# Eight columns instead of four in each group of a four-pass matmul order (gated scan and ELU feed-forward, fp32r)

## The reference

```
f = lower_bound + (1.0 - lower_bound) * sigmoid(f_logit)
i = 1.0 - f
for t in range(S):                       # S = 6080
    h = f[:, t] * h + i[:, t] * x[:, t]
    y[:, t] = h
h = y.reshape(B * S, 256) @ w_in         # 256 x 2048
g = where(h > 0, h, exp(min(h, 0)) - 1)
out = g @ w_out                          # 2048 x 256
```

## Time and profile before

| | before |
|---|---|
| median of 3 runs | 976.56 us |
| the profiled execution, its own time | 976.51 us |
| its span, from the first to the last instruction | 974.6 us |
| matmuls (PE) | 969.0 us busy, 4362 instructions |
| weight loads (PEld) | 815.1 us busy, 4362 instructions |
| VectorE (DVE) | 724.4 us busy |
| ScalarE (ACT) | 790.7 us busy |
| GpSimd (POOL) | 630.6 us busy |
| granted TensorE clock | 1.00 (2.4 GHz) |

### The profile page before, as it was taken

One profiled execution on the slowest core, in us unless ns is written; L12 is line 12 of the kernel. 1 busy time (PEld: TensorE's weight loads), 2 busy tenths in 40 slices (PEclk: granted clock), 3 DMA queues, 4 the chain that ended last, 5 costly groups with the idle time before them and its releaser, 6 DMA issues.

```text
span 974.6 us, 15016 instructions
## 1 busy us (share of the span) xinstructions
PE 969.0 (99%) x4362; PEld 815.1 (84%) x4362; DVE 724.4 (74%) x916; ACT 790.7 (81%) x1424; POOL 630.6 (65%) x477
## 2 busy tenths in 40 slices
PE   9999999999999999999999999999999999999998
PEld 6998888888888888888888888888888888888887
DVE  6987876976886796697688679678758867956444
ACT  7988878878888887887887888788788788787775
POOL 2587796576667667557656755856775765676544
PEclk9999999999999999999999999999999999999999
DMA  7212012002101201100210210120021021001001
GB/s 269 67 32 93 0 34 65 34 1 77 54 1 54 76 1 43 54 32 2 74 54 0 65 65 0 45 67 17 22 64 43 0 75 54 0 0 46 1 1 44
DMA packets 23078, 42.02 MB, mean 43 GB/s; under 512 B 2560, under 2 KB 4096, under 8 KB 23040
## 3 DMA queue, kind: packets, MB, share of 16 engines
q1 hardware_dynamic: 22752, 41.10, 13.1%
q10 hardware_dynamic: 288, 0.46, 0.2%
HBM read 29.10 MB, written 12.45 MB: 43 GB/s over the span
## 4 chain that ended last, share of the span: by engine, by line
PE 99%; DMA 0%; DVE 0%; ACT 0%; issue 0%; DVEq 0%
PE acc L898 17%; PE acc L897 17%; PE acc L899 17%; PE h L868 14%; PE h L867 14%; PE h L866 14%; PE h L1004 1%; PE h L1003 1%; PE h L1002 1%; DMA opening<-first_gate 0%; PE h L969 0%; PE h L979 0%; PE acc L1002 0%; PE acc L1003 0%; PE acc L1004 0%; DVE x L628 0%
## 5 line engine op out<-in xcount | busy, mean ns | idle before, releaser
L336 POOL TENSOR_TENSOR g_lo<-e,g_hi 128x512 fp32r<-128x512 f32 (+1 forms) x384 | 517.3, 1357 | 338.0 <-ACT g_hi L480 337.0
L466 ACT ACTIVATE e<-h 128x512 f32<-128x512 f32 (+1 forms) x379 | 225.1, 594 | 138.5 <-PE h L868 109.9
L719 DVE SCALAR_TENSOR_TENSOR e<-e,h 128x512 f32<-128x512 f32 (+1 forms) x379 | 256.6, 677 | 70.5 <-ACT e L472 69.8
L897 PE MATMUL acc<-g_hi,w_out_hi 128*128 128x512 f32 (+1 forms) x768 | 293.7, 382 | 0.0
L898 PE MATMUL acc<-g_lo,w_out_hi 128*128 128x512 f32 (+1 forms) x768 | 293.7, 382 | 0.0
L899 PE MATMUL acc<-g_hi,w_out_lo 128*128 128x512 f32 (+1 forms) x768 | 293.7, 382 | 0.0
L472 ACT ACTIVATE e<-e 128x512 f32<-128x512 f32 (+1 forms) x384 | 241.4, 629 | 9.8 <-issue 1.4
L480 ACT CAST g_hi<-e 128x512 fp32r<-128x512 f32 (+1 forms) x384 | 232.2, 605 | 18.3 <-DVE e L719 18.3
L866 PE MATMUL h<-a_hi,w_in_hi 128*128 128x512 f32 x616 | 236.6, 384 | 0.0
L868 PE MATMUL h<-a_hi,w_in_lo 128*128 128x512 f32 x616 | 236.6, 384 | 0.0
L867 PE MATMUL h<-a_lo,w_in_hi 128*128 128x512 f32 x616 | 236.5, 384 | 0.0
(11 more groups left out here) (77 smaller groups left out, 560.3 us busy)
## 6 DMA issues: line engine op xcount, KB each, us to landing
opening<-forget_logit SPq DMA_DIRECT2D x44, 256.0 KB, 2.6
x<-value SPq DMA_DIRECT2D x44, 256.0 KB, 2.7
out<-out_sb SPq DMA_DIRECT2D x44, 256.0 KB, 2.0
w_in_raw<-w_in SPq DMA_DIRECT2D x8, 256.0 KB, 5.4
w_out_raw<-w_out SPq DMA_DIRECT2D x8, 256.0 KB, 6.7
out<-out_sb SPq DMA_DIRECT2D x4, 224.0 KB, 2.0
x<-value SPq DMA_DIRECT2D x3, 224.0 KB, 6.0
opening<-forget_logit SPq DMA_DIRECT2D x2, 224.0 KB, 6.0
```

The costliest lines, as they stand in the source:

```text
L336: nc.gpsimd.tensor_tensor(g_lo[:, t % RING, 0:w], e[:, t % TILES, 0:w], g_hi[:, t % RING, 0:w].bitcast(F32), ALU.subtract).then_inc(g_lo_r ...
L466: nc.scalar.activation(e[:, i, 0:w], bank_of(j, t)[:, 0:w], ACT.Relu, scale=-1.0).then_inc(r_ready, 1)
L719: nc.vector.scalar_tensor_tensor(e[:, t % TILES, 0:w], e[:, t % TILES, 0:w], -1.0, bank_of(j, t)[:, 0:w], ALU.add, ALU.max).then_inc(g_rea ...
L897: nc.tensor.matmul(bank, hi, g_h, start=opens, stop=False)
```

## The change

The number of columns of a group goes from four to eight. The four passes stay, so a pass now takes columns 0 to 7, 32 to 39, 64 to 71, ..., the next 8 to 15, 40 to 47, and so on: 4 passes x 16 groups x 8 columns. The row holds the same 512 columns (2048 bytes) as before; a group is 32 bytes in place of 16, and the distance between the groups of a pass is 128 bytes in place of 64.

```
-LINE = 4
+LINE = 8
 APART = 4
 ...
 def in_order(columns):
     return columns.rearrange("p (b a c) -> p a b c", a=APART, c=LINE)
```

## The result

The changed kernel takes **963.62 us** (median of 4 runs, 963.19 to 963.72) against 976.59 us (976.37 to 976.63) of the kernel before. The ratio is 0.9867, with a 95% interval of 0.985 to 0.9884: 1.3% faster. The forecast was 989.7 us, slower, with a range of 966 to 1005 us. The time lies outside the range, and the direction was wrong.

The account below looks back on a forecast made before the run. TensorE was taken as the bound, without idle time. The profiled 976.5 us plus 3960 matmuls at 3.3 ns more each, 13.2 us, gave 989.7 us (+1.35%), with an 8-in-10 range of 966 to 1005 us.

Parts of the forecast that it names:

- What bounds the kernel: Whole kernel: TensorE has no idle time, so time changes by 3960 times the change of one distance between matmul starts.
- The upper end: Blocks 1 to 11: the new distance is bounded above by straight order's 230.0 ns, +6.7 ns a matmul, +26.4 us.
- Steps to the neighbouring group cost: Blocks 1 to 11: 64 of 127 steps go to neighbouring 16-byte groups, losing half the gain: +3.3 ns, +13.2 us; chance 0.30.
- The rival "no change": Blocks 1 to 11: the new order keeps 223.3 ns a matmul, 976.5 us within 0.2%; chance 0.27.
- The rival "faster": Blocks 1 to 11: 64 fewer jumps at 0.060 ns each, −3.8 ns a matmul, −15.2 us, 961.3 us; chance 0.23.
- The rival "all lost": Blocks 1 to 11: weight-load conflict returns, distance as in straight order, 230.0 ns, +26.4 us, 1002.9 us; chance 0.20.
- The 448-column stretch: Block 0: its 202.7 ns distance is near the 187 ns of a weight load, so may be bound by that.
- The rules: Memory rules: SBUF's makes groups of four and eight equal, 976.5 us; PSUM's favours fewer jumps; the trace was put above both.

Follow-up runs that it names:

- e1: Changed kernel with all matmuls of blocks 1 to 11 in straight order, 512 columns from first to last: 989.59 us.
- e8: Changed kernel with 36 series of 24 matmuls of 512 columns behind its end, each in one order, fp32r or bf16: 1167.39 us in all.
- e5: Changed kernel with groups of 8 in four passes on the moving row only, output written in straight order: 963.38 us.
- e6: Changed kernel with the moving row read in straight order and only the output in groups of 8 in four passes: 990.00 us.
- e7: Changed kernel with 64 bytes of room ahead of the rounded rows, so the moving rows begin 64 bytes further on: 989.15 us.
- e11: Changed kernel with the rounded rows put 512 bytes further on, a control for the shift by 64 bytes: 963.74 us.
- e9: Changed kernel with 28 series of 36 matmuls behind its end: fewer weight columns, other groups and passes, shifted moving rows: 1197.46 us in all.
- e14: Changed kernel with one extra matmul of 256 columns just before the first matmul of block 2: 1002.66 us.
- e2: Changed kernel with groups of 16 columns in four passes, 31 jumps: 1040.80 us.
- e4: Changed kernel with groups of 8 columns in two passes in place of four, 63 jumps: 1012.46 us.
- e3: Changed kernel with groups of 8 columns in eight passes in place of four, 63 jumps: 1016.74 us.

## Why the prediction was wrong

**What bounds the kernel: right.** TensorE without a gap, no instruction moved, cost = 3960 x the change of one distance. Span and distance agree within 0.5 us.

**The upper end: off.** 230.0 ns for the straight order came from eight distances in the opening. As a steady stream it has 226.7 ns (e1); a fresh series has more at first, 24 matmuls of e8 give (5.64 − 0.38) / 23 = 229 with their beginning. That the stretch was short stood in the text; the number was used all the same.

**"Steps to the neighbouring group cost": the step that failed.** It made the new order an interpolation between two known ones, 3.3 ns above groups of 4. The measured distance is 3.3 ns below them, 220.0 and not 226.6 ns. Groups of 16 have still more such steps than groups of 8 and should have been between them and the straight order; they have 239.5 ns, 12.8 above it. Groups of 8 in two and in eight passes have just as many as in four and run at 232.4 and 233.3. The distance is no monotonic function of group, jumps or passes: it goes with the order in which the moving row is read (e5, e6), with where the row begins (e7, e11), and with how the stream came in (e9, e14). An interpolation over an unknown mechanism was a guess, and the chances gave it too much.

**The rival "no change"** fell with a difference of 13 us.

**The rival "faster" had the size** (961.3 us, by 0.060 ns a jump) **and not the reason.** Two other orders with the same 63 jumps have 232.4 and 233.3 ns, bf16 in groups of 8 pays nothing for the 63 jumps, and fewer jumps (e2) cost more. Its agreement with 963.6 us is a coincidence. Of its chance of 0.23, the prediction gave 0.13 to a gain beyond the range, and that is where the result lies.

**The rival "all lost"** forecast 1002.9 us, on the ground of a conflict with the weight load. The kick (e14) lands at 1002.66 us, a coincidence as well; the ground, a price that goes with the length of the load, fell with the 32 weight columns of e9. But the direction isn't safe: the same kernel has a distance at which the change would be a loss of 26 us.

**The 448-column stretch** was set aside as perhaps bound by the weight load. It wasn't (194 ns in groups of 8), and so a gain of 1.8 us in block 0 was overlooked.

**The rules.** The Trainium skill, "SBUF — State Buffer", section "Door 1: The DMA port swizzle", says that accesses within a line of 16 bytes run at full bandwidth if there are at least two, and that each step to a new line costs. Groups of 4 to 64 columns all read whole lines and make 127 such steps, so by it they are equal. They run at 220 to 280 ns (280 for groups of 4 in sixteen passes, e8): the rule doesn't tell them apart. The Trainium skill, "PSUM — Partial Sum Buffer", section "Specifications (TRN2)", says that any non-contiguous pattern slows matmuls significantly. With only the output in 4 x 16 x 8, the kernel takes 990.00 us against 989.59 in straight order: no run here shows that slowing.

**What stays open.** Which part of the memory or of the read path is met twice, and so why this order is the better one. It is on the side of the moving reads, depends on the address (64 bytes matter, 512 don't), and is not proportional to the weight load. A row that goes to another 16 bytes 63 times showed none of it. Why the kernels settle at 220.0 and 223.3 ns and not at the other distances of their orders isn't known either, so each distance of e1 to e4 may be one of several. Whether the weight reads take part at all isn't settled: their duration changed with the order (197 ns in e3), and series with shifted weights had other distances, but since an order can have two steady distances, those series don't tell a shift from a state.

## What to carry to other kernels

When TensorE has no gap, read the distance between starts, not the duration, and compare it with a bf16 stream of the same columns (215.7 ns for 512 here): what is above it is neither columns nor waits. The order and the base address of the moving row can be worth several per cent, weren't to be had by interpolation here, and are cheap to try in a series of 36 matmuls. But confirm each in the whole kernel, and look whether one odd matmul in the stream moves it to another steady distance: here one of 0.12 us cost 39 us.

## What the runs showed of the hardware that was unexpected

- fp32r matmuls of 512 columns, 128 x 128 weights, granted clock 2.4 GHz, no waits: 220.0, 223.3, 226.7, 232.4, 233.3 or 239.5 ns by the order in which the moving row is read, as whole kernels. The order of the output made no difference (963.38 and 963.62 us; 990.00 and 989.59 us).
- One order can hold two distances, 220.0 and 230.7 ns, for hundreds of microseconds; in the kernel one matmul of 256 columns switched, one of 448 didn't. Groups of 4 had 223.3 ns in kernels and 227 or 224 in series.
- A shift of the moving rows by 64 bytes: 220.0 to 226.7 ns. By 512 bytes: none.
- Weight loads of 32 columns in place of 128 leave the distance at 247 ns in groups of 4 with eight passes.
- bf16 over 1024 bytes: 216 ns straight and in groups of 8, but 229 in groups of 4; over 2048 bytes: 226 and 220; over 4096 bytes, in groups of 4: 433.
